# A linear-attention and two-layer MLP kernel on one core: scan a cycle sooner, r products on GpSimd, bonuses and the last head pair by other means, output terms two steps behind across passes

## The reference

```python
for t in range(S):
    cur = einsum('bhd,bhe->bhde', u * k[t], v[t])
    y[t] = einsum('bhd,bhde->bhe', r[t], state + cur)
    state = w[t][..., None] * state + einsum('bhd,bhe->bhde', k[t], v[t])
x = y, heads joined                       # 3072 tokens x 384
h = x @ w_in;  x = (h * clip(h + 3, 0, 6) / 6) @ w_out          # 384 -> 2048 -> 384
xn = x / rms(x) * rms_g
out = (silu(xn @ w_gate) * (xn @ w_val)) @ w_out2               # 384 -> 1536 -> 384
```

## Time and profile before

| | |
|---|---|
| median of 3 runs | 991.99 us (988.43 to 994.91) |
| the profiled execution | 993.68 us, span 991.9 us |
| PE busy | 945.7 us, 95% of the span |
| DVE, ACT, POOL busy | 543.2, 363.5, 270.4 us |
| mean granted TensorE clock | 0.979 of full |

### The profile page before, as it was taken

One profiled execution on the slowest core, in us unless ns is written; L12 is line 12 of the kernel. 1 busy time (PEld: TensorE's weight loads), 2 busy tenths in 40 slices (PEclk: granted clock), 3 DMA queues, 4 the chain that ended last, 5 costly groups with the idle time before them and its releaser, 6 DMA issues.

```text
span 991.9 us, 17547 instructions
## 1 busy us (share of the span) xinstructions
PE 945.7 (95%) x7104; PEld 795.2 (80%) x7104; DVE 543.2 (55%) x795; ACT 363.5 (37%) x772; POOL 270.4 (27%) x234
## 2 busy tenths in 40 slices
PE   5768889999999999999999999999999999999998
PEld 5668778888788888888888888888888888888887
DVE  5678676765675667661477453454453454453432
ACT  2455444444344534433646313213213213213212
POOL 3556333433433434332435102101102101102000
PEclk8699999999999999999999999999999999999999
DMA  8365433222322322200432101001001001000000
GB/s 228 97 190 150 121 86 98 84 56 75 97 75 62 111 60 83 71 18 8 144 92 87 38 1 60 5 1 60 5 1 58 7 1 55 9 1 24 9 1 32
DMA packets 33088, 60.99 MB, mean 61 GB/s; under 512 B 6000, under 2 KB 19824, under 8 KB 33008
## 3 DMA queue, kind: packets, MB, share of 16 engines
q1 hardware_dynamic: 26672, 50.69, 17.1%
q10 hardware_dynamic: 6336, 9.18, 3.2%
HBM read 48.24 MB, written 9.44 MB: 58 GB/s over the span
## 4 chain that ended last, share of the span: by engine, by line
PE 88%; issue 1%; DVE 0%; POOL 0%; ACT 0%; ACTq 0%; DVEq 0%
PE acc L963 34%; PE bank L947 11%; PE bank L949 11%; PE bank L948 11%; PE pair L948 5%; PE pair L947 5%; PE pair L949 5%; PE pair L1042 2%; PE pair L1000 1%; PE pair L1033 1%; PE bank L1021 1%; PE bank L1010 1%; POOL gs L860 0%; DVE state L673 0%; PE bank L1111 0%
## 5 line engine op out<-in xcount | busy, mean ns | idle before, releaser
L963 PE MATMUL acc<-gs,w_dn 128*128 128x512 f32 (+1 forms) x1656 | 378.8, 375 | 3.2 <-POOL gs L860 1.9
L963 PEld LDWEIGHTS acc<-gs,w_dn 128*128 128x128 f32 x1656 | 293.2, 190 | 58.9 <-POOL gs L860 3.0
L860 POOL TENSOR_TENSOR gs<-act_g,gs 128x512 fp32r<-128x512 f32 (+1 forms) x112 | 137.2, 1225 | 288.7 <-ACT gs L493 288.6
L947 PE MATMUL bank<-xs,w_up 128*128 128x512 f32 (+1 forms) x480 | 179.2, 373 | 9.9 <-DVE state L673 4.5
L949 PE MATMUL bank<-xs,w_up 128*128 128x512 f32 (+1 forms) x480 | 177.8, 370 | 0.0
L948 PE MATMUL bank<-xs,w_up 128*128 128x512 f32 (+1 forms) x480 | 177.8, 370 | 0.0
L706 DVE SCALAR_TENSOR_TENSOR act_g<-act_u,bank 128x512 f32<-128x512 f32 (+1 forms) x112 | 68.1, 608 | 129.2 <-ACT act_u L485 127.2
L773 DVE TENSOR_TENSOR act_u<-act_u,bank 128x512 f32<-128x512 f32 x72 | 49.5, 688 | 151.4 <-ACT act_u L551 151.3
L485 ACT ACTIVATE act_u<-bank,half 128x512 f32<-128x512 f32 (+1 forms) x112 | 69.8, 623 | 152.8 <-PE bank L949 152.6
L947 PEld LDWEIGHTS bank<-xs,w_up 128*128 128x128 f32 x480 | 91.6, 191 | 26.6 <-DVE state L673 5.5
L949 PEld LDWEIGHTS bank<-xs,w_up 128*128 128x128 f32 x480 | 91.7, 191 | 15.3
(11 more groups left out here) (112 smaller groups left out, 1085.5 us busy)
## 6 DMA issues: line engine op xcount, KB each, us to landing
rkt<-in_rkT SPq DMA_DIRECT2D x48, 192.0 KB, 3.6
rkn<-in_rkN SPq DMA_DIRECT2D x22, 384.0 KB, 3.1
val<-in_valN SPq DMA_DIRECT2D x22, 256.0 KB, 2.8
dec<-in_decT SPq DMA_DIRECT2D x48, 97.5 KB, 2.2
x<-x_dram SPq DMA_DIRECT2D x6, 768.0 KB, 4.3
x_dram<-xo SPq DMA_DIRECT2D x5, 768.0 KB, 5.0
out<-xo SPq DMA_DIRECT2D x5, 768.0 KB, 3.3
raw<-in_w_out ACTq DMA_DIRECT2D x17, 192.0 KB, 2.4
```

The lines of the kernel that those rows point to most:

```text
L860: pool.tensor_tensor(gs[:, f % GRING, 1, tok], act_g[:, f % 2, tok], gs[:, f % GRING, 0, tok].bitcast(F32), ALU.subtract).then_inc(s_glo, 1)
L947: pe.matmul(dst, w_hi, x_hi, start=first, stop=False)
L963: last = pe.matmul(ps_o[m][:, tok], w[:, wp, m * P:(m + 1) * P], gs[:, f % GRING, xp, tok], start=f == 0 and a == 0, stop=f == nf - 1 and ...
```

## The change

- **The cycle.** `prep_scan(g+3)` and the reciprocals of g+3 run in group g's phases, one group sooner than before; `prep_k(g+2)` moves from INV2 to PREP. Since cum of g is then overwritten before the state is scaled by its last column, `keep_last` copies that column (112x8) to a ring. `scale_state` moves out of update_state, from MEET to PREP. sum_bonus moves to INV1. Loads of the decays go one group further ahead.
- **r products.** `prep_r` moves from DVE to POOL, after g_lo of the PREP step. For all groups.
- **Bonuses of groups 0 and 1.** POOL multiplies r by k in the transposed layout (`rk_mul`), TensorE multiplies by u laid out per head (`bonuses`, u_h, 4 matmuls of 2 columns per group), ACT copies the result. Their natural-layout loads of r and k are gone.
- **Last pair of groups 0 and 1.** ACT copies the last two heads of v into a zero-padded tile val3 (`place_val3`), and 12 matmuls of 64 columns (`inside3`) add them to the x1 rows at once. The fold matrix, its 6 matmuls per group, and the raw copy are gone.
- **Passes.** `down(14)` and `down(15)` of a pass run inside steps 0 and 1 of the next; x2_out moves to step 1, after the attention work; `down(0)` waits for x2_out. MEET of group 3 moves from step 12 of pass 0 to 11.
- **The start.** The ACT table load comes before the weight loads; busy matmuls go from 34 to 26; fill_bonus(2) moves into steps 0 and 1; u_b is loaded later, by SP.

```diff
 def prep_scan(g):
     need(dve, s_ki, g - 1)
-    state_taken(dve, g - 2)
+    need(dve, s_rd, g - 1)
...
-def prep_r(g):                                      # on DVE
+def keep_last(g):
+    dve.wait_ge(s_cum, g + 1)
+    dve.tensor_copy(last[0:DP, g % LASTS, :], cum[0:DP, slot(g), :, :, T:T1].rearrange("p a b t -> p (a b t)")).then_inc(s_last, 1)
...
 def attention(phase, g, par):                       # DVE
     if phase == MEET:
         if has_state(g):
             update_state(g)
-        x1_lo(g, par)
+        if g >= PLACED:
+            x1_lo(g, par)
...
     if phase == PREP:
-        if prep < GROUPS:
-            prep_scan(prep)
-            prep_r(prep)
-            sum_bonus(prep)
-    if phase in (INV1, INV2) and prep < GROUPS:
-        prep_inv(prep, phase - INV1)
-        if phase == INV2:
-            prep_k(prep)
+        if has_state(g) and not is_first(g):
+            scale_state(g)
+        if g + 2 < GROUPS:
+            prep_k(g + 2)
+        if g + 3 < GROUPS:
+            prep_scan(g + 3)
+            keep_last(g + 3)
+    if phase == INV1 and g + 2 < GROUPS:
+        sum_bonus(g + 2)
+    if phase in (INV1, INV2) and g + 3 < GROUPS:
+        prep_inv(g + 3, phase - INV1)
...
+def rk_mul(g):                                      # POOL
+    landed(pool, ldR, g, 2)
+    r_in, k_in = (rkt[0:DP, g, i, :, :, :].rearrange("p a b t -> p a (b t)") for i in range(2))
+    pool.tensor_tensor(rk_t[g][0:DP, :, :], r_in, k_in, ALU.mult).then_inc(s_rkt, 1)
+def prep_r(g):
+    landed(pool, ldR, g, 2)
+    pool.wait_ge(s_cum, g + 1)
+    need(pool, p_y, g - 1)
+    pool.tensor_tensor(... rd <- rkt r, cum ..., ALU.mult).then_inc(s_rd, 1)
+def attention(phase, g):
+    if phase == MEET and g + 2 < GROUPS:
+        rku_mul(g + 2)
+    if phase == PREP and g + 2 < GROUPS:
+        prep_r(g + 2)
...
 def down(e, f):                                     # PE
     pe.wait_ge(s_glo, e * NF1 + f + 1)
+    if f == 0:
+        need(pe, s_x2, KT * e)
...
+def inside3(g, k):
+    for b, j in TILES:
+        last = pe.matmul(y_of(g)[HI2 * j:HI2 * (j + 1), b, k * T:(k + 1) * T], val3[T * b:T * (b + 1), g, j, k, :],
+                         att[T * b:T * (b + 1), g, j, PAIRS - 1, :], start=False, stop=True, skip_group_check=True)
+def bonuses(g):
+    pe.wait_ge(ldH, 16)
+    pe.wait_ge(s_rkt, g + 1)
+    for p in range(PAIRS):
+        last = pe.matmul(bonus_bank(g)[:, 2 * p:2 * p + 2], rk_t[g][0:DP, p, :], u_h[0:DP, p, :], start=True, stop=True)
...
 def run1(...):                                      # PE, a pass
         if f >= 2:
             down(e, f - 2)
+        elif e:
+            down(e - 1, NF1 - 2 + f)
...
-    down(e, NF1 - 2)
-    if nxt_par is not None:
-        up(e + 1, 0, nxt_par)
-    down(e, NF1 - 1)
...
 def run1(...):                                      # ACT, a pass
         up_gate(e, f)
-        if f == 0:
-            x2_out(e - 1)
...
         g_hi(e, f)
         for phase, g in steps.get(f, ()):
             attention(phase, g, par)
+        if f == 1:
+            x2_out(e - 1)
```

More of the change, by code:

```diff
@@ L110, in build @@
         y3 = sa("y3", [P, 2, C], F32R)
-        fold = xo[:, :, 0:P]
-        y3_raw = xo[:, 0, P:P + C]
+        val3 = sa("val3", [P, PLACED, 2, KT, HI2])
+        u_h = sa("u_h", [P, PAIRS, 2])
+        last = sa("last", [P, LASTS, PAIRS * PB])
+        rk_t = [xo[:, g, :].rearrange("p (a t) -> p a t", a=PAIRS) for g in range(PLACED)]
         upper = att[:, 0, 0, 0:2, :].rearrange("p a t -> p (a t)")
@@ L243, in build @@
                   7: [(MEET, 2)], 8: [(PREP, 2)], 9: [(INV1, 2)], 10: [(INV2, 2)],
-                  12: [(MEET, 3)], 13: [(PREP, 3)], 14: [(INV1, 3)]}
+                  11: [(MEET, 3)], 12: [(PREP, 3)], 13: [(INV1, 3)]}
         def slot_up(j):
@@ L363, in store_x2, with attention @@
                     sp.dma_start(x2_dram[e - 1], xo[:, :, :]).then_inc(stX, 16)
+            def attention(phase, g, par):
+                if phase == MEET:
+                    move_y3(g, par)
+                if phase == PREP and g + 2 < GROUPS:
+                    load_val(g + 2)
+                if phase == INV1:
+                    if g + 5 < GROUPS:
+                        load_dec(g + 5)
+                    if g + 4 < GROUPS:
+                        load_rk(g + 4)
+                if phase == INV2 and g + 4 < GROUPS:
+                    load_rkn(g + 4)
             def run1(e, steps, par):
@@ L367, in run1 @@
                     for phase, g in steps.get(s, ()):
[L368 to L380, removed]
+                        attention(phase, g, par)
+                    if s == 1:
+                        store_x2(e - 1)
             for g in range(2):
@@ L890, in run1 @@
                     for phase, g in steps.get(f, ()):
-                        if phase == MEET and g + 2 < GROUPS:
-                            rku_mul(g + 2)
+                        attention(phase, g)
                     if norm:
@@ L1049, in outputs @@
                 pe.wait_ge(s_mask, g + 1)
[L1050 to L1055 removed]
+                if g < PLACED:
+                    pe.wait_ge(s_val3, g + 1)
                     for p in range(PAIRS - 1):
                         inside(g, p)
[L1058 removed]
                     for k in range(KT):
[L1060 to L1062 removed]
+                        last = inside3(g, k)
                     last.then_inc(p_y, 1)
                     return
+                need(pe, s_x1lo, 2 * g)
                 for p in range(PAIRS):
@@ L1138, in busy @@
                 for _ in range(n):
-                    pe.matmul(ps_c[:, 0:P], ones[:, :].bitcast(F32), ones[:, :].bitcast(F32), start=True, stop=True)
+                    pe.matmul(ps_o[0][:, 0:P], ones[:, :].bitcast(F32), ones[:, :].bitcast(F32), start=True, stop=True)
             pe.wait_ge(s_ones, 1)
-            busy(34)
+            busy(26)
+            bonuses(0)
             pe.wait_ge(const, NCONST)
```

262 lines of the change are left out of this document (123 added, 139 removed).

## The result

| | before | after |
|---|---|---|
| median | 992.52 us (988.43 to 994.91, 4 runs) | 966.82 us (965.63 to 967.42, 4 runs) |
| profiled execution | 993.68, span 991.9 | 967.0, span 965.2 |
| mean granted clock | 0.979 | 0.988 |

A forecast was written before the change was run, and what follows sets the result against it. PE, busy 95% of the span, was taken as bound, losing time in the first 166 us and at pass boundaries, mainly waiting for DVE's ki. Terms -10.1 - 8.3 - 12.0 - 3.2 = -33.6 gave 959 us, range 944 to 977.

The forecast's parts named there:

- unnamed wait: PE idling 15.1 us in seven places before scores matmuls, listed only as "issue"; claimed to be for DVE's ki.
- A: Prologue, 38.09 us to the first `up`: claimed -10.1 us, bounds -7 to -13.
- Rival 2: Prologue keeps its length because ACT's queue or r and k landing sets x1: A about -2, 967; chance 0.08.
- B: Pass 0, first `up` to scores in step 1 of pass 1, 65.88 us: claimed -8.3, bounds -14 and 0.
- Rival 1: Shared SBUF ports keep DVE the bound: B 0, C only -6, 973 us; chance 0.13.
- C: Pass 1, 61.96 us: waits before scores and for the state end; claimed -12.0 us, bounds -6 to -14.
- D: 512-token passes: the 0.80 us state wait in four is covered by a `down`; claimed -3.2, bounds -4 to +4.
- Rivals 3: From pass 0 the granted clock stays at 1.2 GHz through PE's many short gaps: slower, 1032 us; chance 0.04.
- Rival 4: Wait before scores stays, rd on POOL coming as late as ki did: A and D only, near 979; chance 0.04.
- rival 5: New waits at the six pass boundaries (x2_out, y3 moves), 1 to 2.5 us each: +9, 968; chance 0.06.
- signs I had named: Profile afterwards: first `up` at 27 to 29, scores near 86 and 136, DVE over 85% busy, rd 1.3 to 1.9 us.
- signs of failure: Prediction fails if POOL's rd exceeds 2.5 us, g_lo is late for its `down`, or half clock lasts past 45 us.

The follow-up runs named there:

- experiment 10: Changed kernel with only ki moved back to INV2, two steps later; 980.33 us.
- experiment 7: Changed kernel with the raw copy and fold matmuls of groups 0 and 1 back in place of val3; 971.9 us.
- experiment 8: Changed kernel with g_hi first in pass 0, r*k*u products in INV2, rd in INV1 from pass 1 on, last-pass norm one step later; 961.11 us.
- experiment 4: Changed kernel with POOL's twelve low weight parts of pass 0 cut from 384 to 16 columns, output not the reference's; 962.5 us.
- experiment 2: Changed kernel with POOL's products moved beside DVE's reciprocals: rd to INV1, r*k*u products of the next group to INV2; 963.65 us.
- experiment 1: Changed kernel with rd (r times cum) of groups 3 to 23 back on DVE; 967.37 us.
- repeated 9: Second run of experiment 8 with the last-k-column copies of groups 4 and up moved from DVE to ACT; 960.83 us.
- experiment 5: Kernel before with the pass boundaries alone changed: down(14) and down(15) in the next pass's steps 0 and 1, x2_out in step 1; 989.13 us.

## Why the prediction was right in its sign and 8 us too low

**What bounds the kernel: right.** All but 4.2 of the 26.7 us came before the scores in step 1 of pass 2. That the unnamed wait is ki's was shown by experiment 10.

**A: right in its size, -9.7 for -10.1, partly by luck.** The scores of group 0 started at 11.63, sooner than my 14.0, because the first scan started at 5.67 (7.94 before). ACT's DMA issues ended at 7.70, where I had 11.5. Both leads were lost: ACT waited for TensorE's bonuses until 11.80, PE's bonus matmuls of group 1 waited 1.08 us for POOL's product of r and k and stood until 15.77, a wait that I hadn't counted, and x1_lo of group 0 started at 18.68, where I had 19.0. x1_lo of group 1 ended at 28.25, where the sum had 27.9. The fold is 5.9 of it (experiment 7). Rival 2 (ACT keeps the prologue long) is out.

**B: the mechanism was named, its size was not.** The step that failed is the last of B: "Add 1.5 for POOL's rd holding up DVE's two-operand instructions". It charged rd alone, and charged it once, while ki, the scaled state, the copies and the weight pieces stood in the sum at what they take beside an idle or half-idle POOL. By stages, with hidden(3), hidden(7) and hidden(11) at 43.60, 59.43 and 75.47, I was off by +1.9 at hidden(3), then +2.1, +0.6, and +1.2 to the scores, 5.8 in all, of which 0.4 is the later start. The first part is another omission: DVE waited 1.96 and 0.56 us for ACT's high parts,

```profile
34.95 1.05 DVE L733 TENSOR_TENSOR w_dn<-raw,w_dn 128x384 fp32r<-128x384 f32 x1 [1.96 <-ACT w_dn L455]
...
38.60 1.04 DVE L733 TENSOR_TENSOR w_dn<-raw,w_dn 128x384 fp32r<-128x384 f32 x1 [0.56 <-ACT w_dn L455]
```

a queue I hadn't followed. The rest is turns: in three cycles ki at 1.38 to 1.50 for the 0.9 or so that I counted (+1.7), the copies at 0.80 to 0.97 for 0.1 each (+2.3), the state at 1.04 for the 0.55 that it takes in experiment 8, twice (+1.0), together 4.9 (of unrounded terms) against the 1.5 allowed, +3.4. With ACT's 2.5 that has the size of the miss, though the third cycle lies where I took PE for the bound, and nothing says that all of it is on the path. That the turns with POOL cost the pass its time is shown (experiment 4), and that ki and the state shrink once POOL works elsewhere (2, 8). What share the low clock from 40 to 48 us has isn't settled: the cycle that holds it took 16.48 us here, 16.50 in experiment 1 at a clock of 1.00 (with rd on DVE), but 15.06 in experiment 8 and 16.37 in the repeated 9, which differ little but in that.

**Rival 1 was half true.** It priced an rd on POOL at all that it frees. B came nearer to its 0 than to my -8.3. Experiment 1 agrees for the passes: moving rd gave 0.5 us. It was wrong in that DVE would then stay the bound before the scores of pass 1; there POOL has pauses, and the wait for ki went whole. The rule of the Trainium skill, page "SBUF — State Buffer", section "Who interferes with whom" (a VectorE instruction with two SBUF inputs and a GpSimd one that reads SBUF shut each other out, and so do a VectorE copy in a two-port mode and a GpSimd instruction) is what the rows show, also in what it exempts: reciprocal and reduction, with one input, stood at 913 and 542 ns throughout; which mode the small copy runs in no row says. I had weighed it for one instruction, and it holds for seven or eight in a cycle of pass 0: the scaled state, ki, the scan, the copy and the weight pieces.

**C: right in its mechanism, 2.0 us short.** No scores wait and no clock dip were left, as said, and x1's wait for the y3 moves came at 1.4 for my 1.1 (the terms I gave add up to 1.3). But POOL's rd still meets DVE's next instructions; experiments 2 and 8, with the products beside the reciprocals, reach 49.55 and 49.54, below my 50.0.

**D: -4.2 for -3.2, with two terms missing.** My sum put at nothing the `down(15)` of pass 1 that moves into D, +1.1, though B's count of 15 `down` had lent one; with it the sum is -32.5. The wait of 0.80 for the state went, as said, and a 512-token pass took 77.68 us (scores at 220.17 and 297.85) for my 78.1. A one-off gap of 1.17 us at 267 us of the kernel before is gone as well, without my having asked for it. I missed that `down(14)` and `down(15)` in the last pass put POOL's squares behind more g_lo: 1.07 us at 474 us. The change of D is within what single runs of the kernel before differ by (6 us), and experiment 5 bounds the boundary change at 1 to 5 us.

**Rivals 3, 4 and 5.** The clock came back by itself: 1.00 from 48 us on (3). Rival 4 is out. Of 5, 1.4 and 1.1 us came true. The measured 966.8 is rival 2's 967 and near rival 5's 968, but neither was the cause.

**The signs I had named.** Met: the first `up` at 28.40 (27 to 29), no wait before scores, DVE busy for 34.69 of the 40 us from 30 to 70 (87%). Missed: the scores at 91.51 and 143.46, for 86 and 136, and an rd on POOL of 2.12 us, for 1.9 at most. Two of my three signs of failure showed in part: one `down` waited 1.34 us for g_lo (at 87.00), and the half clock lasted to 48 us (0.54 from 46 to 48), not 45.

## What to carry to other kernels

Here work moved from VectorE to GpSimd freed VectorE only where it ran while VectorE did one-input instructions or waited; so before costing such a move, list what both engines will do in that phase, and count every two-input VectorE instruction and every copy at its stretched duration. Here the placement of the same products (beside the reciprocals) gave more (3.2 us, experiment 2) than the move itself (0.5, not clear of noise, experiment 1). What gave most was order: ki made two steps sooner, with the engines' work unchanged, was worth 13 us (experiment 10); the scan and reciprocals have to run a group ahead for that.

## What the runs showed of the hardware that was not expected

- For an instruction that waits its turn, size counts for little. A DVE copy of 112x8 took 0.17 us alone and 0.80 to 0.97 beside POOL; a 128x16 difference took 578 ns in the mean, the 128x384 one 963.
- Both sides pay. POOL's rd took 1.18 us alone and 1.58 to 2.12 beside DVE; g_lo of 128x256 took 0.74 and up to 1.75 (experiment 4); a 128x16 piece 0.22, and 0.61 and 0.67.
- The scan takes turns too: 1.23 us alone, 1.77 with g_lo beside it, 2.23 with rd beside it (experiment 4, at 76.83 us), where the copy behind it then took 0.17 again.
